# Sums of squares on ScalarE, one cast per pair, and first-layer units regrouped in a two-mixture kernel

## What is computed

```python
def reference(**kwargs):
    attn_out = _attn_ref(q, k, v, w_phi)                  # 4 x 8 heads, 576 rows, width 64
    x = attn_out.transpose(0, 2, 1, 3).reshape(2304, 512)
    x = _moe_ref(x, w_gate, w1, w2)
    return _moe2_ref(x, expert_emb, tau, w1b, w2b)

def _moe_ref(x, w_gate, w1, w2):                          # 2304 rows, 8 experts, 512 -> 1024 -> 512
    P = ...                                               # normalised gates, 8 sweeps
    for e in range(8):
        out += P[:, e:e+1] * (np.maximum(x @ w1[e], 0) @ w2[e])
```

## Time and profile before

| | |
|---|---|
| median of 2 runs | 2353.06 us (2352.75 to 2353.37) |
| profiled execution | 2346.36 us, its span 2344.5 us |
| busy share of the span | PE 86%, DVE 70%, ACT 38%, POOL 21% |
| mean granted TensorE clock | 0.951 |

### The profile page before, as it was taken

How to read it: one execution, slowest core, us unless ns; L and a number is a source line. 1 busy time by engine, 2 the same in 40 slices (tenths; PEclk the granted TensorE clock), 3 DMA queues, 4 the chain that set the end, 5 groups by cost and what they waited for, 6 DMA issues and landing times.

```text
span 2344.5 us, 45908 instructions
## 1 busy us (share of the span) xinstructions
PE 2024.1 (86%) x17514; PEld 1696.6 (72%) x17514; DVE 1646.7 (70%) x3287; ACT 893.0 (38%) x1755; POOL 481.2 (21%) x310
## 2 busy tenths in 40 slices
PE   6968978789689878979987898889789999699998
PEld 5757867677568767867776687778677888566765
DVE  7847887788677777777767767877777775734343
ACT  3535433334334344434433343443344443222221
POOL 0633842300320230041004102300410000111211
PEclk9979979899899989999998999999999999889999
DMA  6132021224222132313312231323132322261420
GB/s 189 36 92 62 21 73 45 73 91 164 71 108 100 46 108 91 136 64 109 109 65 91 100 118 46 112 88 136 63 109 77 116 106 82 95 265 42 177 97 11
DMA packets 123162, 221.73 MB, mean 95 GB/s; under 512 B 63542, under 2 KB 63670, under 8 KB 121792
## 3 DMA queue, kind: packets, MB, share of 16 engines
q1 hardware_dynamic: 111888, 183.62, 22.9%
q10 hardware_dynamic: 7056, 25.69, 3.2%
q0 software_dynamic: 4000, 9.45, 1.3%
HBM read 151.88 MB, written 70.52 MB: 95 GB/s over the span
## 4 chain that ended last, share of the span: by engine, by line
PE 53%; DVE 23%; issue 11%; ACT 5%; DMA 4%; POOL 3%; SPq 0%; DVEq 0%; ACTq 0%; POOLq 0%
PE ps L950 17%; PE ps L927 16%; PE ps L1111 6%; DVE arena L1556 4%; PE ps L1095 4%; DVE wg L1414 4%; DVE arena L1631 3%; PE ps L876 3%; DVE arena L1568 2%; DMA arena<-in_moe_w_dram 2%; DVE arena L1559 2%; PE ps L1097 2%; DVE arena L1558 2%; PE ps L889 2%; ACT arena L1193 2%
## 5 line engine op out<-in xcount | busy, mean ns | idle before, releaser
L950 PE MATMUL ps<-arena 128*128 128x256 f16 x6048 | 769.9, 281 | 214.1 <-DVE arena L1631 197.7
L950 PEld LDWEIGHTS ps<-arena 128*128 128x128 f16 x6048 | 595.6, 101 | 340.4 <-DVE arena L1631 211.0
L927 PE MATMUL ps<-arena 128*128 128x256 f16 x6912 | 808.3, 273 | 5.7 <-ACT arena L1231 5.1
L927 PEld LDWEIGHTS ps<-arena 128*128 128x128 f16 x6912 | 677.8, 98 | 87.2 <-ACT arena L1231 6.4
L1231 ACT ACTIVATE arena<-ps 128x256 f32<-128x256 f32 x576 | 206.9, 377 | 574.1 <-PE ps L927 563.0
L1568 DVE TENSOR_TENSOR arena<-arena 128x384 f16<-128x384 f32 x576 | 383.8, 667 | 4.3 <-ACT arena L1238 3.5
L1240 ACT ACTIVATE arena<-arena 128x512 f16<-128x512 f32 x288 | 181.4, 630 | 426.1 <-DVE arena L1561 426.1
L1631 DVE SCALAR_TENSOR_TENSOR arena<-ps,wt,arena 128x256 f32<-128x256 f32 x441 | 211.5, 480 | 155.3 <-PE ps L950 152.8
L1556 DVE TENSOR_TENSOR arena<-arena 128x128 f32<-128x128 f32 x288 | 142.0, 493 | 190.2 <-ACT arena L1231 189.2
L602 POOL PARTITION_ALL_REDUCE wm<-wg x32 | 12.2, 380 | 816.9 <-DVE wg L1414 766.6
L720 POOL TENSOR_TENSOR arena<-arena 128x1024 f16<-128x1024 f32 x49 | 106.9, 2186 | 312.3 <-ACT arena L1180 305.2
(11 more groups left out here) (213 smaller groups left out, 1893.8 us busy)
## 6 DMA issues: line engine op xcount, KB each, us to landing
arena<-in_moe_w_dram SPq DMA_DIRECT2D x16, 2048.0 KB, 9.0
split_weights<-arena SPq DMA_DIRECT2D x64, 512.0 KB, 3.0
arena<-in_moe_w_dram SPq DMA_DIRECT2D x64, 512.0 KB, 4.9
arena<-split_weights SPq DMA_DIRECT2D x8, 4096.0 KB, 13.6
second_weights<-arena SPq DMA_DIRECT2D x49, 512.0 KB, 3.2
arena<-second_weights ACTq DMA_DIRECT2D x49, 512.0 KB, 3.7
arena<-in_q_dram SPq DMA_DIRECT2D x16, 288.0 KB, 3.6
arena<-in_k_dram SPq DMA_DIRECT2D x16, 288.0 KB, 4.0
```

Source lines behind the costliest of these rows:

```text
L927: last = pe.matmul(o, ring[:, slot, sw, FF * c + 128 * j:FF * c + 128 * j + 128], xT[:, sx, c, BLK * blk:BLK * blk + BLK], start=(i == 0), ...
L950: last = pe.matmul(region(n, u), hop[:, u, sh, p, o, :], w2op[:, o, sw, p, :], start=(i == 0 and k in (0, 1, 3)), stop=(i == 3 * Q - 1), s ...
```

## The change

Four things change in the first mixture.

- The third and fourth pair of units (n = 4 to 7) both stand behind product 2, where the fourth stood behind product 3 (`BEHIND`). VectorE's accumulations are placed anew (`READS`).
- For pairs 0 to 2 the seven operands are cast by one instruction and subtracted by one (896 columns); pair 3 keeps two of each.
- The measure of a weight's size is no longer its largest value, from VectorE, but the sum of squares of each quarter row, from ScalarE (`bound`); the maximum over these goes on as before, and the scale is worked out from its halved exponent.
- The hooks move. On ScalarE, for pairs 0 to 2, they stand between the relus and the cast; on VectorE the scale stands ahead of the sums, and the lower parts stand behind the pair.

```diff
+HALVES = Q + 1
...
         FRESH = (0, 2, 3, 6)
+        BEHIND = ((0, 1), (2, 3), (4, 5, 6, 7), (), (), (), ())
+        READS = ((1,), (2,), (), (3, 4))
         PIECES = (A11, A12, S4, S1, S3, S2, A22)
...
                         u = PLANS[plan]["order"].index(job) % 2
-                        across(wm[:, u, :], wg[:, u, :], RMAX, wmax_done, n + 1, wall_done)
+                        across(wm[:, u, :], wg[:, u, :], RMAX, bound_done, WP * (n - 1), wall_done)
...
                 if k == 0:
-                    pe.wait_ge(hlo_done, FC * (ub + 1) - 1)
+                    pe.wait_ge(hlo_done, HALVES * (ub + 1) - 1)
                 if k == 2:
-                    pe.wait_ge(hlo_done, FC * (ub + 1))
+                    pe.wait_ge(hlo_done, HALVES * (ub + 1))
                 free = OPS * ub + {0: 0, 1: 6 - OPS, 2: 1, 3: 2, 4: 3, 5: 4, 6: 5}[k]
...
                                 last_rows(k)
-                            for n in range(2 * k, 2 * k + 2 if k < Q and not end else 2 * k):
+                            for n in BEHIND[k] if not end else ():
                                 if blk < NB - 1:
...
                 act.wait_ge(h1_done, FC * ub + n + 1)
-                if x == 0 and due(FC * ub + n - 2):
-                    act.wait_ge(hlo_done, FC * ub + n - 2)
+                if x == 0:
+                    read = HALVES * ub + p - 1 if p > 1 else HALVES * (ub - 1) + 3 + 2 * p
+                    if due(read):
+                        act.wait_ge(hlo_done, read)
                 dst = tb[:, p % 2, 1:3, :] if x else tb[:, p % 2, 0:S3 + 1:S3, :]
...
                     act.wait_ge(y_done, OPS * (ub - 1))
-                act.activation(hop[:, u, 0, p, 0:3, :], tb[:, p % 2, 0:3, :], ACT.Copy).then_inc(hhi_done, 1)
+                o0 = 0
+                if p == Q - 1:
+                    act.activation(hop[:, u, 0, p, 0:3, :], tb[:, p % 2, 0:3, :], ACT.Copy).then_inc(hhi_done, 1)
+                    o0 = 3
                 act.wait_ge(hsum_done, 4 * (Q * ub + p + 1))
-                act.activation(hop[:, u, 0, p, 3:OPS, :], tb[:, p % 2, 3:OPS, :], ACT.Copy).then_inc(hhi_done, 1)
+                act.activation(hop[:, u, 0, p, o0:OPS, :], tb[:, p % 2, o0:OPS, :], ACT.Copy).then_inc(hhi_done, 1)
+
+            def bound(plan, par, e, job, k):
+                n = number(plan, e, job)
+                done, value = loads(plan, e, job)
+                u = PLANS[plan]["order"].index(job) % 2
+                if k == 0:
+                    act.wait_ge(done, 16 * value)
+                    act.wait_ge(wall_done, n - 1)
+                seen = WP * (n - 2) + k - 1
+                if due(seen):
+                    act.wait_ge(bound_done, seen)
+                act.activation(spent[:, k % 2, :], raw_of(plan, par, job)[:, WPC * k:WPC * k + WPC], ACT.Square,
+                               accum_out=wg[:, u, k:k + 1]).then_inc(bound_done, 1)
+
+            def weights_hook(plan, c, par, e, h):
+                if h in PLANS[plan]["top"]:
+                    job, k0 = PLANS[plan]["top"][h]
+                    for k in (k0, k0 + 1):
+                        bound(plan, par, e, job, k)
+                for job, k in PLANS[plan]["hi"].get(h, ()):
+                    cut_hi(plan, c, par, e, job, k)
...
                                     copy_rows(ROWS[blk, n])
+                            if p < Q - 1:
+                                weights_hook(plan, c, par, e, Q * blk + p)
                             operands_hi(ub + 1, (par + blk + 1) % 2, p)
...
                                    .then_inc(sk_exp, 1)
-                            for job, k in PLANS[plan]["hi"].get(Q * blk + p, ()):
-                                cut_hi(plan, c, par, e, job, k)
+                            if p == Q - 1:
+                                weights_hook(plan, c, par, e, Q * blk + p)
                             if plan != "last" and blk == NB - 1:
...
                 dve.wait_ge(wscale_done, 4 * n + 1)
-                scale_of(wscale_done, 4 * n + 1, wsc[:, at, 0:1], wsc[:, at, 3:4], inv)
+                if isinstance(n, int) and n < 2:
+                    scale_of(wscale_done, 4 * n + 1, wsc[:, at, 0:1], wsc[:, at, 3:4], inv)
+                    return
+                bits = inv.bitcast(i32)
+                dve.tensor_scalar(bits, wsc[:, at, 0:1].bitcast(i32), 1, EXPMASK, ALU.arith_shift_right, ALU.bitwise_and)\
+                   .then_inc(wscale_done, 1)
+                dve.wait_ge(wscale_done, 4 * n + 2)
+                dve.tensor_scalar(inv, inv, 2.0 ** (64 - TOP), 2.0 ** -(56 + TOP), ALU.mult, ALU.max).then_inc(wscale_done, 1)
+                dve.wait_ge(wscale_done, 4 * n + 3)
+                dve.reciprocal(wsc[:, at, 3:4], inv).then_inc(wscale_done, 1)
+                dve.wait_ge(wscale_done, 4 * n + 4)
...
-            def weights_hook(plan, c, par, e, h):
-                if plan == "second" and h == 0:
-                    cut_lo("first", 0, 0, 0, "B1", WP - 1)
-                if h in PLANS[plan]["top"]:
-                    job, k0 = PLANS[plan]["top"][h]
-                    done, value = loads(plan, e, job)
-                    u = PLANS[plan]["order"].index(job) % 2
-                    for k in (k0, k0 + 1):
-                        largest(number(plan, e, job), u, raw_of(plan, par, job), k, done, value)
+            def scale_hook(plan, par, e, h):
                 if h in PLANS[plan]["scale"]:
...
                                           inv, 1.0, None, ALU.mult)
+
+            def weights_hook(plan, c, par, e, h):
+                if plan == "second" and h == 0:
+                    cut_lo("first", 0, 0, 0, "B1", WP - 1)
                 for job, k in PLANS[plan]["lo"].get(h, ()):
...
-            def operands_lo(ub, u, p, x):
-                some = slice(0, 3) if x == 0 else slice(3, OPS)
-                dve.wait_ge(hhi_done, FC * ub + 2 * p + x + 1)
-                if x == 1:
+            def operands_lo(ub, u, p, x=None):
+                some = slice(0, OPS) if x is None else slice(0, 3) if x == 0 else slice(3, OPS)
+                dve.wait_ge(hhi_done, HALVES * ub + p + 1 + (x or 0))
+                if x != 0:
                     dve.wait_ge(hsum_done, 4 * (Q * ub + p + 1))
...
                         for p in range(Q):
+                            scale_hook(plan, par, e, Q * blk + p)
+                            operand_sums(ub + 1, p)
+                            if p == Q - 1:
+                                operands_lo(ub + 1, 1 - u, p, 0)
+                            for k in READS[p]:
+                                accumulate(e, blk, ub, k, plan, u)
+                            operands_lo(ub + 1, 1 - u, p, 1 if p == Q - 1 else None)
+                            if p == Q - 1:
+                                accumulate(e, blk, ub, 5, plan, u)
+                                accumulate(e, blk, ub, 6, plan, u)
                             if plan == "first":
...
                                 early_table(blk, p)
-                            operand_sums(ub + 1, p)
-                            operands_lo(ub + 1, 1 - u, p, 0)
-                            accumulate(e, blk, ub, p + 1, plan, u)
-                            operands_lo(ub + 1, 1 - u, p, 1)
-                        for k in (5, 6):
-                            accumulate(e, blk, ub, k, plan, u)
                         if plan == "last":
```

8 lines of the change are left out of this document (5 added, 3 removed).

## The result

The changed kernel takes 2657.86 us (median of 2 runs, 2656.39 to 2659.34) against 2353.06 us, 1.1295 times the time before, 95% interval [1.1247, 1.1344]. The forecast was 2490 us with a range of 2400 to 2580: slower, as forecast, but by 305 us where I had worked out 142.

What follows compares the result with a forecast made beforehand. TensorE waits on VectorE's accumulation chain, which has nothing to spare in a quiet block; 114 us of new waits plus 28 of clock make 142 on 2346.4, 2488 us, called 2490, range 2400 to 2580.

Steps and rivals of the forecast that it cites:

- part 2: VectorE's lower parts behind the pair: 1.2 us each directly before pair 3's sums, 4.8 us in block 7.
- the terms of blocks 2 and 3: Product 5's lateness in a middle expert: 5.6 to 10.4 us in block 2, 2.8 to 4.6 in block 3.
- GpSimd's holds: VectorE's small sums held during GpSimd's two-tensor subtractions: all remain; one between units 4 and 5 and product 5 costs up to 2.2 us more.
- block 1: ScalarE's weight cast, now ahead of pair 2's cast, waits for GpSimd's scaling; product 5 comes 6.2 to 9.5 us late.
- Part 1: Units 6 and 7 behind the third product, one cast per pair: quiet blocks 0.63 us longer, room per pair 1.29 to 0.75.
- The quiet block: A block that nothing disturbs, 20.48 us before, becomes 0.63 us longer, 21.1 us, as pair 3's sums start late.
- block 0: In a middle expert, squares behind pair 2 and the scale before pair 3 make product 5 2.4 us late.
- Block 7: Four lower parts behind pairs 0 and 1 of a middle expert: product 5 4.8 us late, block 25 us.
- Part 3: Squares on ScalarE at 1.1 us each: two delay the cast by 1.0 us; VectorE loses 120 reductions, 140 us busy.
- The rival in which VectorE's load decides: Stalls come from VectorE's queued work, 140 us of which goes: faster, 2288 us; chance 0.08.
- The clock: Idle time lowers the granted clock, 0.25 us for each us idle: 114 us of new waits bring 28 more.
- everything adds: Rival: holds meet the chain at the high end and a square costs 1.3 us: 2550 to 2620 us; chance 0.08.

Runs made afterwards that it cites:

- a_old_hooks: Changed kernel with upper parts of weights behind the cast and lower parts ahead of the sums again, squares still ahead of the cast; 2488.64 us (1.0598).
- b_regroup: Kernel before with only the units regrouped: units 4 to 7 behind product 2, accumulations 3 and 4 at pair 3; 2444.07 us (1.0409).
- b_regroup_reads: Kernel before with units 6 and 7 behind the third product, but the third accumulation left at pair 2; 2393.43 us (1.02).
- b_cast_group: Kernel before with the single cast and subtraction for pairs 0 to 2 and the new order of units, reductions and lower parts as before; 2553.04 us (1.0871).
- a_hooks_behind: Changed kernel with ScalarE's upper parts of weights and the squares both moved behind the pair's cast; 2639.18 us (1.1239).
- b_squares: Kernel before with only the squares on ScalarE, behind the casts, in place of VectorE's reductions; 2369.86 us (1.0097).
- b_squares_ahead: Kernel before with only the squares on ScalarE, ahead of the casts of pairs 0 to 2, old plan; 2322.69 us (0.9898).
- b_one_cast: Kernel before with only one cast and one subtraction for pairs 0 to 2, reductions still on VectorE; 2443.09 us (1.0403).
- a_all_back: Changed kernel with weight hooks and units as before, leaving the single cast and the squares ahead of the cast; 2377.15 us (1.0122).
- a_units_back: Changed kernel with units 6 and 7 behind product 3 again and accumulations as before, casts and hooks as changed; 2521.19 us (1.0736).

## Why the prediction was right in sign and wrong in size

**The main failure is in part 2 and in the terms of blocks 2 and 3.** I moved the lower parts and the upper parts each in its own queue and priced both as lengths of work there: 2.48 us for two lower parts, 5.6 to 10.4 us of lateness in block 2, 2.8 to 4.6 in block 3, the spread only from GpSimd's holds. Measured in expert 3: 17.27 and 11.12, plus 1.40 before units in block 3; together 29.8 us where the forecast's ends were 8.4 and 15.0. What I did not follow, and so put at nothing, is the loop through the transfer: lower part, transfer out of the staging buffer, next upper part. The trace before had it with slack, as the lower part went first and the upper part last. With the hooks back in their places (a_old_hooks) the wait for the buffers is gone and the two blocks idle 7.25 and 5.15 us, inside my range for block 2 and 0.55 above it for block 3. What both moves cost together is 169 us, more than the whole of my 142; not all of it is the loop, since in expert 3 the move also brought 5.8 us into block 1, where I had forecast it. Over the five middle experts the idle time grew by 35 us each where the sum had 16, and blocks 2 and 3 hold nearly all of the difference. For experts 0 and 1 the estimates of 15 and 10 us were short too (29 and 31 us); no run takes those two apart.

**Part 1 was right where it was worked out and wrong where it was carried over.** The quiet block, 0.63 us from both parts together, came out within 0.01 us (21.12, and 20.48 with either part alone). For disturbed blocks I took over the idle times of before and added the room that pairs lose. b_regroup and b_regroup_reads show the missing term: product 5 inherits the date that product 6 had, 1.31 us earlier, in every block in which VectorE is late, about five of nine. The order alone cost 97 us where I had nothing, the single cast 96 where I had its 0.54 us only in pairs already late.

**That block 0 came out is partly luck.** The move of the date, which I had left out, and the squares, which I had counted as a delay, cancel: block 0 of expert 3 idles 4.58 us in b_cast_group, with the reductions, and 2.15 in a_old_hooks and in the changed kernel, with the squares ahead of the cast; I had 2.4. By time, part 1 alone costs 206 us (b_cast_group).

**Block 1 was right.** The wait for GpSimd's scaling came as told: 4.56 us before L1184 at 1145.85, and product 5 9.71 us late, just above the high end of 6.2 to 9.5. Block 7 too (27.73 us; 4.42 of idle for 4.8), block 0 (2.15 for 2.4), block 4 (4.22 for 3.6 to 5.4), blocks 5, 6 and 8 (2.87, 2.27, 0.55 for 3.2, 2.3, 0.6).

**Part 3 had the right duration and the wrong sign.** I took 1.1 us for a square; the step is 1.04. I counted two squares ahead of a cast as 1.0 us of delay. In a_hooks_behind and in b_squares against b_squares_ahead that place is the better one by 56 and 47 us, since behind the cast the squares delay the next relus. The rival in which VectorE's load decides expected 2288 us from all of the change; made alone and in its best place this part gives 24 us (0.9898 [0.9872, 0.9924]), and b_one_cast against a_all_back shows that it is worth 66 us once VectorE has no room. It is worth as much with the new order of the units: b_cast_group and a_old_hooks differ only in it, and take 2553.04 and 2488.64 us, 64 us apart. No run shows what it is worth together with the moved hooks.

**GpSimd's holds** stood as forecast: VectorE's first sum fell only from 493 ns to 409, and part of what it lost moved to the subtraction of 896 columns, whose mean is 1261 ns against 1.09 us undisturbed. Counted over the rows of the stage, 66 of VectorE's sums and subtractions are longer by 0.25 us and more beside a GpSimd subtraction, before and after alike. In block 2 the holds now meet the chain four times in a row, 2.28 to 2.70 us each. That is the trace's answer to the rule that I had cited from the Trainium skill (GPSIMD Engine Reference, Specifications): the two agree.

**The clock.** TensorE's idle time grew by 246 us (436.9 and 28.4 before products and units, by the groups by line, against 214.1 and 5.7) and the stage by 308.5, so 63 us are clock: 0.26 us for each us of idle time, with 0.25 forecast. That this fits is in part luck, for the price isn't constant from run to run: the stage of b_regroup is 97.0 us longer than before with 61.5 more of idle time on TensorE, 0.58 us for each, and that of a_units_back 174.7 with 162.2, 0.08 for each.

**The signs that I named**: product 5 waits and not product 6, quiet blocks at 21.1, the weight cast in block 1 released by GpSimd's scaling were all there. Block 7 took 27.73 for 25 us, since its 4.42 us of idle time brought a clock of 0.88 with it. The idle time before products by the accumulations was to be near 300 us and is 378.2. The stage grew by 167 us more than my sum of 142: 132 are idle time that I hadn't counted (246 for 114) and 35 the clock that came with it (63 for 28).

**The range** failed with its high case: I gave "everything adds" 0.08 and let it end at 2620, with bounds for blocks 2 and 3 that had no room for a wait of another kind.

## What to carry to other kernels

When a step is moved in an in-order queue, follow its result round the whole loop to the buffer that it frees, through the other engine and the transfer: a producer moved late on one engine and a consumer moved early on another cost 95 and 74 us here, and TensorE, which neither move touched, did the waiting. When work that another engine reads is regrouped, ask for every reader which instruction now releases it and how much earlier its date is; price this in the blocks that are already late, where slack does not hide it, not in the quiet one. Extra work for an engine that waits anyway belongs inside that wait (the squares ahead of the cast, while VectorE sums), not behind the last thing that others wait for: the same 120 instructions, each in place of a reduction on VectorE, cost 23 us in the one place and gave 24 us in the other.

## What the runs showed of the hardware

A square with its sum over the row leaves two records on ScalarE, 1.04 us for 1024 columns and a second of 0.19 us that reads the accumulator; the next instruction starts 1.04 us after the square did, so the second costs nothing beside a plain cast of 1024 columns (1.04 us). Four GpSimd subtractions in a row (2.12, 2.52, 2.40, 2.49 us) each held one VectorE instruction that began beside them and ended 0.15 to 0.95 us behind them, a subtraction of 896 columns (2.28 us instead of 1.09) as well as a sum of 128 (2.42 instead of 0.29).
